# Inverse sums of a pair of heads handled within one round of the DMA queue, and a subtraction moved from GpSimd to VectorE

## What is computed

```
q_rot, k_rot = rotate(q), rotate(k)
scores = scale * q_rot @ k_rot^T
attn = exp(scores - max(scores)); attn = attn / (sum(attn) + 1e-9)
x = (attn @ v), heads joined: 2304 x 512
for w_in (512 x 2048), w_out (2048 x 512) of layers 1 and 2:
    h = x @ w_in
    g = h - tanh(h)                  # layer 1
    g = h * (1 / (1 + exp(-h)))      # layer 2
    x = g @ w_out
```

## Time and profile before

| | |
|---|---|
| runs | 1101.76, 1104.51, 1107.02 us; median 1104.51 |
| the profiled execution | 1107.88 us, its span 1106.0 us, mean granted clock of TensorE 0.991 |
| TensorE (PE) busy | 1064.7 us, 96% of the span |
| VectorE (DVE) busy | 435.3 us, 39% |
| ScalarE (ACT) busy | 412.1 us, 37% |
| GpSimd (POOL) busy | 282.8 us, 26% |
| attention, to the first feed-forward matmul | the first 298 us |
| chain that ended last | PE 82%, DMA 8% |

### The profile page before, as it was taken

One profiled execution on the slowest core, in us unless ns is written; L12 is line 12 of the kernel. 1 busy time (PEld: TensorE's weight loads), 2 busy tenths in 40 slices (PEclk: granted clock), 3 DMA queues, 4 the chain that ended last, 5 costly groups with the idle time before them and its releaser, 6 DMA issues.

```text
span 1106.0 us, 18105 instructions
## 1 busy us (share of the span) xinstructions
PE 1064.7 (96%) x7404; PEld 997.6 (90%) x7404; DVE 435.3 (39%) x696; ACT 412.1 (37%) x760; POOL 282.8 (26%) x127
## 2 busy tenths in 40 slices
PE   3889999989999999999999999999999999999998
PEld 2879888879999999999999999899989989899897
DVE  5556666656252323232232333523223232322322
ACT  2557776666722323223232322323223232232322
POOL 6667897966470000000000015700000000000000
PEclk9999999999999999999999999999999999999999
DMA  5445455453151000000000004200000000000000
GB/s 194 161 140 157 143 147 179 143 160 84 38 188 52 1 1 0 0 0 0 0 0 0 0 0 152 77 1 28 0 0 28 0 28 0 0 28 0 28 0 29
DMA packets 36368, 60.54 MB, mean 55 GB/s; under 512 B 15712, under 2 KB 18016, under 8 KB 34400
## 3 DMA queue, kind: packets, MB, share of 16 engines
q1 hardware_dynamic: 36320, 59.87, 17.0%
HBM read 50.46 MB, written 4.79 MB: 50 GB/s over the span
## 4 chain that ended last, share of the span: by engine, by line
PE 82%; DMA 8%; SPq 3%; POOL 3%; DVE 2%; ACT 1%; issue 1%; ACTq 0%; POOLq 0%; DVEq 0%
PE ps L722 35%; PE ps L741 18%; PE ps L736 17%; DMA inverse_sums<-rinv 4%; PE ps L592 3%; PE ps L556 2%; PE ps L586 2%; DMA R<-inverse_sums 2%; DMA sums<-ev 1%; PE ps L496 1%; PE ps L622 1%; SPq L282 1%; DVE hm L919 1%; POOL xT L412 1%; PE ps L546 1%
## 5 line engine op out<-in xcount | busy, mean ns | idle before, releaser
L722 PE MATMUL ps<-xs_h,win_l 128*128 128x384 f32 x768 | 258.6, 337 | 1.4 <-DVE xs_l L979 1.4
L722 PE MATMUL ps<-xs_h,win_h 128*128 128x384 f32 x768 | 257.6, 335 | 0.0
L722 PE MATMUL ps<-xs_l,win_h 128*128 128x384 f32 x768 | 257.1, 335 | 0.0
L884 ACT ACTIVATE g_h<-ps 128x384 fp32r<-128x384 f32 x192 | 94.4, 492 | 306.1 <-PE ps L741 135.1
L878 ACT ACTIVATE act<-ps 128x384 f32<-128x384 f32 x192 | 94.5, 492 | 247.7 <-PE ps L722 247.6
L722 PEld LDWEIGHTS ps<-xs_h,win_l 128*128 128x128 f32 x768 | 144.2, 188 | 7.5 <-issue 3.9
L722 PEld LDWEIGHTS ps<-xs_l,win_h 128*128 128x128 f32 x768 | 144.2, 188 | 3.5
L722 PEld LDWEIGHTS ps<-xs_h,win_h 128*128 128x128 f32 x768 | 144.1, 188 | 0.0
L919 DVE TENSOR_REDUCE hm<-ps 128x2 f32<-128x576 f32 x144 | 108.5, 756 | 63.4 <-PE ps L496 56.8
L736 PE MATMUL ps<-g_h,wout_h 128*128 128x384 f32 x384 | 128.3, 334 | 0.0
L736 PE MATMUL ps<-g_h,wout_l 128*128 128x384 f32 x384 | 128.3, 334 | 0.0
(11 more groups left out here) (86 smaller groups left out, 1619.6 us busy)
## 6 DMA issues: line engine op xcount, KB each, us to landing
raw<-qk SPq DMA_DIRECT2D x15, 1152.0 KB, 5.9
w_stage<-w_in SPq DMA_DIRECT2D x8, 1024.0 KB, 5.0
w_stage<-w_out SPq DMA_DIRECT2D x8, 1024.0 KB, 5.2
v<-vfull SPq DMA_DIRECT2D x16, 384.0 KB, 4.1
R<-inverse_sums SPq DMA_DIRECT2D x32, 144.0 KB, 3.1
out<-ostage SPq DMA_DIRECT2D x5, 768.0 KB, 3.5
vr<-vin SPq DMA_DIRECT2D x16, 192.0 KB, 3.2
ev<-ev SPq DMA_DIRECT2D x16, 144.0 KB, 2.3
```

The costliest lines, as they stand in the source:

```text
L722: last = mm(o, w[g][:, kk, c:c + 128], x[:, kk, :], start=(n == 0), stop=(n == 11))
L884: nc.scalar.activation(g_h[f % 2][:, :], ps[:, 4 + f % 4, 0:TN], ACT.Copy, scale=(1.0, 0.5)[L]).then_inc(s_gh, 1)
```

## The change

Round n of SyncE's loop now handles the sums of pair n - 1 from the gathering to the spreading. Before, it gathered and joined those of pair n - 1 and stored and spread those of pair n - 2. VectorE inverts before the low part of unit 7, not at the end of the pair. The low part of v for the next pair is taken by VectorE right behind the inversion; GpSimd no longer takes it. Buffers, DMAs and their sizes are the same.

```diff
--- before.py
+++ after.py
@@ -342,30 +342,29 @@
             for n in range(PAIRS):
                 if n + 3 < PAIRS:
                     load(n + 3)
-                if n >= 2:
-                    store_inverse(n - 2)
                 if n + 1 < PAIRS:
                     load_split_v(n + 1)
-                if n >= 2:
-                    spread_inverse(n - 2)
+                if n >= 1:
+                    gather_sums(n - 1)
                 if 1 <= n < PAIRS - 1:
                     load_full_v(n + 1)
                 if n >= 1:
-                    gather_sums(n - 1)
                     join_heads(n - 1)
+                    store_inverse(n - 1)
                 if n + 1 < PAIRS:
                     max_rows(n + 1)
+                if n >= 1:
+                    spread_inverse(n - 1)
                 if n + 2 < PAIRS:
                     sp.wait_ge(s_lq, n + 3)
                     copy_blocks(n + 2, slice(0, 4), s_bd[n % 2])
                 if n in W_LOAD:
                     load_w(W_LOAD[n])
-            for n in (PAIRS - 2, PAIRS - 1):
-                if n == PAIRS - 1:
-                    gather_sums(n)
-                    join_heads(n)
-                store_inverse(n)
-                spread_inverse(n)
+            n = PAIRS - 1
+            gather_sums(n)
+            join_heads(n)
+            store_inverse(n)
+            spread_inverse(n)
             for w in range(4, 4 * NG):
                 load_w(w)
             for t in range(NT - 1):
@@ -399,12 +398,6 @@
                 pool.wait_ge(s_hq, n + 1)
                 nc.gpsimd.tensor_tensor(t[:, QL:KL + 1:2, 0:S], raw[n % 2][:, 0:2, :],
                                         t[:, QH:KH + 1:2, 0:S].bitcast(F32), ALU.subtract).then_inc(s_lq, 1)
-
-            def v_low(n):
-                a, b = vh[n % 2], vl[n % 2]
-                pool.wait_ge(s_vh, n + 1)
-                nc.gpsimd.tensor_tensor(quarters(b)[:, :, 0:4:3, :], vr[:, :, :, :], quarters(a)[:, :, 0:4:3, :].bitcast(F32),
-                                        ALU.subtract).then_inc(s_vl, 1)
 
             def normalise(n):
                 pool.wait_ge(s_mv, 16 * (n + 1))
@@ -444,19 +437,14 @@
                 pool.wait_ge(t, 16)
             rope_scale(1)
             rope_add(1)
-            v_low(0)
             qk_low(1)
             rope_scale(2)
             rope_add(2)
             for n in range(PAIRS):
                 if n + 2 < PAIRS:
                     qk_low(n + 2)
-                if n == 0:
-                    v_low(n + 1)
                 if n + 3 < PAIRS:
                     rope_scale(n + 3)
-                if n and n + 1 < PAIRS:
-                    v_low(n + 1)
                 if n + 3 < PAIRS:
                     rope_add(n + 3)
                 if n in W_QUARTER:
@@ -941,6 +929,12 @@
                 dve.wait_ge(s_re, n + 1)
                 nc.vector.reciprocal(rinv[:, :], rinv[:, :]).then_inc(s_ri, 1)
 
+            def v_low(n):
+                a, b = vh[n % 2], vl[n % 2]
+                dve.wait_ge(s_vh, n + 1)
+                nc.vector.tensor_tensor(quarters(b)[:, :, 0:4:3, :], vr[:, :, :, :], quarters(a)[:, :, 0:4:3, :].bitcast(F32),
+                                        ALU.subtract).then_inc(s_vl, 1)
+
             for t in hl:
                 nc.vector.memset(t[0:64, :, S + 64:COLS].bitcast(F32), 0.0)
                 nc.vector.memset(t[64:128, :, S:S + 64].bitcast(F32), 0.0)
@@ -988,6 +982,8 @@
             for j in range(8):
                 row_max((0, j), XB if j == 7 else (XB, 2)[j % 2])
             row_max((0, 9), 2)
+            dve.wait_ge(s_cst, 8)
+            v_low(0)
             for n in range(PAIRS):
                 x_place(n, "S0")
                 low(9 * n)
@@ -998,9 +994,11 @@
                 x_place(n, "S4", "B1", "S5")
                 low(9 * n + 5)
                 x_place(n, "S6", "S7")
+                invert(n - 1)
+                if n + 1 < PAIRS:
+                    v_low(n + 1)
                 low(9 * n + 7)
                 x_place(n, "S8", "A5")
-                invert(n - 1)
             n = PAIRS - 1
             invert(n)
 
```

## The result

The changed kernel takes 1120.29 us (median of 4 runs, 1118.66 to 1121.17) against 1103.13 us (4 runs, 1101.09 to 1107.02): a ratio of 1.0152, 95% interval 1.0129 to 1.0176. The forecast was 1105 with a range up to 1118, so the result lies above it. The profiled execution took 1118.66 us (span 1116.9).

The account below looks back on a forecast made before the run. TensorE needs 14.7 us per pair; anything above is stalls, in long pairs from late R. Ordinary pairs +4.7, long pairs -5.0, pair 1 +0.3 sum to 0.0 us: 1105 us on the median's scale, range 1092 to 1118.

Parts of the forecast that it names:

- The failed step: VectorE's low part of v, ahead of the low part of unit 7: 557 ns, alone a 0.3 us stall per pair, not added.
- The row maxima behind the store: SyncE issues the next pair's row maxima behind the inverse's store: TensorE's scores stall 1.2 us per pair, pairs 2 to 13.
- R a pair earlier: R issued at the end of SyncE's round n: GpSimd's wait of 56.5 us mostly goes, ScalarE's for xT goes.
- The copies: Copies of the diagonal blocks stand behind R in SyncE's queue: 0.2 us per pair, between nothing and 0.6.
- v behind the weights: In pairs 2, 9, 12 v's load follows weights and q/k: TensorE stalls 2.9 us, clock adds 1.3; three pairs total 60.3.
- Rival B: The clock falls at every new TensorE gap of 1.2 us between pairs: +11, 1116 us; chance 0.30.
- The scale: Sum of 0.0 made against the profiled execution of 1107.88 us; the median is 3.4 lower, giving 1105 us.

Follow-up runs that it names:

- run 8: The kernel before, unchanged, profiled a second time: 1101.47 us in one execution.
- run 1: The changed kernel with the low part of v back on GpSimd, new queue order and earlier inversion kept: 1108.56 us, ratio 1.0048 against the kernel before.
- run 2: The changed kernel with one wait added: GpSimd's second scaling waits until VectorE's subtraction of v is done: 1109.64 us, ratio 1.005 against the kernel before.
- run 10: New queue, subtraction on GpSimd, row maxima and block copies ahead of the store, weights a round later, v's load ahead of q and k: 1086.09 us.
- run 4: The changed kernel with v's low part back on GpSimd and the rows of maxima issued ahead of the inverse's store: 1109.38 us, ratio 1.0058.
- run 3: The kernel before with only v's low part moved to VectorE, queue and inversion as they were: 1104.16 us, ratio 1.001.

## Why the prediction was wrong, point by point

Periods in sums, from the marks of each kernel (us):

| | nine ordinary pairs | pairs 2, 9, 12 | time of that execution | median |
|---|---|---|---|---|
| before, profile of the prediction | 140.2 | 65.3 | 1107.88 | 1103.13 |
| before, profiled again (run 8) | 138.7 | 58.6 | 1101.47 | |
| forecast | 144.9 | 60.3 | | 1105 |
| without the VectorE part (run 1) | 146.1 | 58.2 | 1106.08 | 1108.56 |
| GpSimd held back (run 2) | 146.4 | 59.8 | 1110.59 | 1109.64 |
| changed kernel | 160.4 | 55.9 | 1118.66 | 1120.29 |
| v first (run 10) | 134.1 | 48.4 | 1085.65 | 1086.09 |

- *The failed step* is "On VectorE a subtraction of 128x384 takes 557 ns ... Alone that is a stall of 0.3 us per pair." It takes 2.9 us, in nine pairs in a row. Put into the prediction's own chain, 2.35 us more make the stall 0.3 + 2.35 = 2.65, which overtakes the 1.2 of the maxima, and a pair takes 17.35; measured are 17.2. The row taken was right for its own operands, one of them in PSUM: such an instruction takes 0.56 us whether GpSimd works or not. The right question would have been which ports the moved instruction reads through, and what GpSimd runs at that moment.
- *The row maxima behind the store: right.* L290 is issued 8.8 us behind the mark, as forecast (151.17 in pair 6, whose mark is 142.36), and runs 1 and 2 have ordinary pairs of 16.2 and 16.3 us in the mean where 16.1 was forecast. In pair 4 of run 1 the next pair's scores start 10.55 us behind the mark (112.24, mark 101.69), where the chain gave 10.56. As idle time of TensorE the stall is 0.8 us, not 1.2, and the period is met by other parts than forecast: in the six pairs of run 1 TensorE is idle for 0.9 us each and busy for 15.2, where the sum has 1.4 and 14.7. The fixed cost in "DMA: Bandwidth & Descriptors" of the Trainium skill, from which the prediction works out 1.4 us, is given there for DMAs that GpSimd issues; here SyncE issues them, and the row of this kernel was nearer. In the changed kernel this stall is hidden under the longer one: TensorE waits for mr<-rows twice only.
- *R a pair earlier: right*, with 21.6 us of GpSimd's waiting left (5 times, up to 9.5) and none of ScalarE's.
- *The copies: right in place, a little larger.* In run 1 TensorE waits for them 3.8 us in 5 times, 1.1 at the longest, which is over the 0.6 us that the prediction set as the limit of its term; in the ordinary pairs it comes to 0.3 us each, where 0.2 was counted. In the changed kernel they show once (1.0 us), since the longer stall hides them, and they cost 11.3 us as soon as the maxima are not late (run 4).
- *v behind the weights: right in size with the subtraction on GpSimd,* 58.2 against 60.3 (run 1), in part by luck: the sum has 1.3 us for the clock in each of the three, and in run 1 the clock is below 1.00 in pair 12 alone (0.91). In the changed kernel itself it is oversized, 55.9: its longer pairs give SyncE time, and in pair 9 v lands before ScalarE comes to it.
- *Rival B, the clock: in part.* In pairs 4 to 7, 10 and 11 a gap of 2.2 us, larger than the 1.2 that the rival spoke of, left the clock at 1.00; in pairs 3, 8 and 9 the mean is 0.84 to 0.91. So B was too pessimistic about each gap, and in runs 1 and 2 all nine ordinary pairs stand at 1.00. The clock is the smaller part, but not nothing: pair 8 is 1.5 us longer than pairs 4 to 7, and pair 3 is 4.3 longer, with a gap of 3.2 us in it, where the held subtraction makes a row maximum late. Without these 5.8 us the time would lie inside the range. They stand behind gaps that the hold makes, and are part of the 11.7 us that run 1 takes off.
- *The scale.* The profile that the sum was made against had 6.7 us more in the long pairs than the second one. Against that one the changed kernel's ordinary pairs cost 21.7 and the long ones gain only 2.7, 19.0 in all. The two spans differ by 17.3 us and the medians by 17.2, so some 1.7 are gained outside those pairs. Most of the 6.7 us is clock: in pairs 2 to 13 TensorE has the lower clock for 17.1 us in the first profile and for 6.8 in the second, and at half the speed half of the 10.2 us between them is lost, 5.1. The prediction took the 65.3 as typical: with 58.6 for the long pairs its own sum would have been 4.7 + 1.5 (ordinary, by 138.7) + 1.7 + 0.3 = +8, which on 1103.13 gives 1111; run 1, the change without the hold, has 1108.56.

Two errors, then, in the same direction: one of about 12 us from the hold, which the runs show, and one of some 5 us (run 1 is 5.4 over the kernel before, where the sum has 0.0), most of which comes from taking a single execution's long pairs as typical. That second reading rests on two profiles only.

## What to carry to other kernels

Before an elementwise instruction is moved between VectorE and GpSimd, look where its inputs lie and what the other engine runs at that moment: with two SBUF inputs, begun beside a GpSimd instruction of 2.6 us, it lost up to 2.4 us, and a periodic kernel may repeat the worst phase in every round. A move that cost nothing in one order of the queue (run 3) cost 12 and 20 us in two others. In an in-order DMA queue, put a load ahead of a store only if the load's own wait does not hang on what the store feeds: the same step was worth 10 to 13 us in one order and cost 44 in another. And when a sum books a gain from a few long stalls, take a second profile before trusting their size.

## What was not expected of the hardware

The hold is not symmetric in its cost: VectorE lost up to 2.4 us (2.91 against 0.50), GpSimd 0.3 (2.98 against 2.67). Each waits for the rest of the other's instruction, and GpSimd's are longer here (2.6 us against 0.5).

The same gap does not always lower the clock. TensorE in stretches of 1 us in the changed kernel, columns as in the earlier trace rows:

```profile
153.00:154.00 1.00, 0.00 (x0) 1.00 0.00 0
...
156.00:157.00 1.00, 1.00 (x18) 1.00 1.39 263
```

```profile
187.00:188.00 1.00, 0.00 (x0) 1.00 0.00 1
...
191.00:192.00 1.00, 1.00 (x10) 0.50 0.71 238
```

The first are of pair 6, the second of pair 8. Both gaps last 2.25 us and end in the same matmuls; after the second the granted clock is 0.50, the lower of the two levels, for 3.4 us, after the first it stays at the higher. No run here tells what decides between them.
